# Moving the norm's weight into the second matrix of an MLP, and centring and scaling rows in one GpSimd instruction

## What is computed

```
x = attention(q, k, v)                      # 2304 x 512
h = x @ w_in                                # 2304 x 1024
sm = exp(h - max(h)) / (sum(exp(h - max(h))) + 1e-9)
solu = h * sm
mu = mean(solu);  var = mean((solu - mu) ** 2)
ln = (solu - mu) / sqrt(var + 1e-6) * g_ln  # g_ln: 1024 weights, one per column
y = ln @ w_out                              # 2304 x 512
out = softplus(y @ w_in2) @ w_out2
```

## Time and profile before

| | before |
|---|---|
| median of 3 executions | 927.47 us (927.47 to 928.46) |
| the profiled execution's own time | 928.05 us |
| its span in the profile | 926.2 us |
| PE busy | 900.5 us, 97% |
| DVE busy | 763.8 us, 82% |
| ACT busy | 499.7 us, 54% |
| POOL busy | 433.0 us, 47% |

### The profile page before, as it was taken

The page is one execution under the profiler, slowest core; times in us unless marked ns, Lnnn a source line. Parts: engine busy times, 40 slices in busy tenths (PEclk is TensorE's granted clock), DMA queues, the critical chain, the costliest instruction groups (busy, mean ns, idle before and its releaser), DMA issues.

```text
span 926.2 us, 15249 instructions
## 1 busy us (share of the span) xinstructions
PE 900.5 (97%) x5456; PEld 745.0 (80%) x5456; DVE 763.8 (82%) x1304; ACT 499.7 (54%) x936; POOL 433.0 (47%) x449
## 2 busy tenths in 40 slices
PE   7999999999999899999999899999999999999997
PEld 4666666666667698898999788899999999999995
DVE  6899998999874938448352799999999999999997
ACT  3777777778764624334342655445445545455543
POOL 3444444345652824123140555555556565556563
PEclk9999999999999999999999999999999999999999
DMA  6713413422210100000000720000000000000000
GB/s 168 204 29 77 104 41 65 103 73 61 65 47 1 42 6 1 1 1 1 1 12 1 233 74 1 35 1 1 35 1 1 35 1 1 34 0 0 34 0 35
DMA packets 29491, 37.58 MB, mean 41 GB/s; under 512 B 3696, under 2 KB 17520, under 8 KB 29424
## 3 DMA queue, kind: packets, MB, share of 16 engines
q1 hardware_dynamic: 29024, 36.42, 14.2%
q10 hardware_dynamic: 400, 0.30, 0.1%
HBM read 31.98 MB, written 4.72 MB: 40 GB/s over the span
## 4 chain that ended last, share of the span: by engine, by line
DVE 50%; PE 44%; issue 4%; ACT 1%; DMA 0%; POOL 0%; DVEq 0%; SPq 0%
DVE g L848 13%; PE y_ps L1042 11%; PE o_ps L978 9%; PE s_ps L940 9%; PE t_ps L951 7%; DVE g_hi L852 7%; DVE g L838 7%; DVE g_lo L854 6%; PE h_ps L909 5%; DVE g L841 5%; DVE x_lo L704 2%; DVE solu L805 1%; DVE ntop L709 1%; DVE st_top L791 1%; DVE ln_lo L767 1%
## 5 line engine op out<-in xcount | busy, mean ns | idle before, releaser
L451 POOL TENSOR_TENSOR w_lo<-w_raw,w_hi 128x512 fp32r<-128x512 f32 x96 | 131.8, 1374 | 161.2 <-ACT w_hi L631 159.1
L412 POOL TENSOR_SCALAR kept<-kept,inv 128x576 f32<-128x576 f32 x144 | 105.9, 751 | 137.4 <-DVE inv L741 137.4
L511 ACT ACTIVATE expd<-s_ps,ntop 128x576 f32<-128x576 f32 x144 | 104.7, 741 | 71.6 <-DVE ntop L709 71.6
L1018 PE MATMUL m_ps<-y_hi,w_lo 128*128 128x384 f32 x384 | 131.2, 342 | 0.0
L1018 PE MATMUL m_ps<-y_lo,w_hi 128*128 128x384 f32 x384 | 130.1, 339 | 0.0
L647 ACT ACTIVATE l<-u 128x384 f32<-128x384 f32 x96 | 50.4, 525 | 146.0 <-POOL u L459 146.0
L1018 PE MATMUL m_ps<-y_hi,w_hi 128*128 128x384 f32 x384 | 128.8, 335 | 0.0
L709 DVE TENSOR_REDUCE ntop<-s_ps 128x1 f32<-128x576 f32 x144 | 106.0, 755 | 23.6 <-PE s_ps L940 17.4
L459 POOL TENSOR_TENSOR u<-z,consts 128x384 f32<-128x384 f32 x96 | 105.8, 1102 | 41.7 <-ACT z L640 41.6
L1099 PE MATMUL f_ps<-w_hi,g_hi 128*128 128x512 f32 x288 | 115.8, 402 | 8.0 <-DVE g_lo L854 8.0
L848 DVE TENSOR_TENSOR g<-g,l 128x384 f32<-128x384 f32 x96 | 119.0, 1239 | 2.8
(11 more groups left out here) (85 smaller groups left out, 1803.7 us busy)
## 6 DMA issues: line engine op xcount, KB each, us to landing
q_sb<-q_t SPq DMA_DIRECT2D x28, 288.0 KB, 5.1
v_sb<-v_main SPq DMA_DIRECT2D x16, 256.0 KB, 3.2
stage<-w_in SPq DMA_DIRECT2D x16, 256.0 KB, 2.7
w_raw<-w_out SPq DMA_DIRECT2D x8, 512.0 KB, 6.5
out<-o_sb SPq DMA_DIRECT2D x5, 768.0 KB, 3.6
k_sb<-k_t SPq DMA_DIRECT2D x21, 144.0 KB, 4.6
stage<-w_in SPq DMA_DIRECT2D x4, 512.0 KB, 8.4
stage<-w_out SPq DMA_DIRECT2D x4, 512.0 KB, 3.6
```

Of the source, the lines that this page charges most:

```text
L412: nc.gpsimd.tensor_scalar(kept[:, tile % RING, :], kept[:, tile % RING, :], inv[:, group % 2, k:k + 1], 1.0, ALU.mult, ALU.mult).then_inc( ...
L451: nc.gpsimd.tensor_tensor(w4[1][:, n % 2, :], w4_raw[:, n % F2, :], f32(w4[0][:, n % 2, :]), ALU.subtract).then_inc(w4lo_made, 1)
L1018: last = nc.tensor.matmul(m_ps[n % 4][:, 0:GC], w[:, k, (n % F2) * P:(n % F2 + 1) * P], y[odd][:, k, :], start=(k == 0 and m == 0), stop=( ...
```

## The change

The norm's weight `g_ln` no longer multiplies the rows of `ln` but the rows of `w2`, once. It is loaded early as 128 x 8 numbers, with weight 128k + p in partition p and column k. In the doubles 72 to 75 of attention, the last ones, ACT multiplies each of the eight row blocks of `w2` in its `stage` slot by its column (`w2_scale`), before it takes the high part. In the first MLP DVE's instruction that made `(solu - mu) * gain` (L820) goes, and POOL's multiplication by `st_rstd` becomes one instruction with two per-partition scalars: `(solu + nmean) * rstd`. As POOL now reads `solu` itself, DVE waits before it writes a `solu` buffer until POOL has read the tile two before, and POOL waits for PE's transposes before it writes `ln`. POOL's loop over tiles is written out. The full diff:

```diff
@@ tensors
+        gain = sb("gain", [P, F1])
...
-        gain = sb("gain", [P, DFF1], where=phase)
@@ sync
                 sp.dma_start(staged(n)[0], staged_source(n)).then_inc(stage_in[n], 16)
+            sp.dma_start(gain[:, :], gain_d.rearrange("(k p) -> p k", p=P),
+                         allow_slow_non_contiguous=True).then_inc(gain_in, 16)
             for unit in range(2, UNITS):
...
-            sp.dma_start(gain[:, :], gain_d.partition_broadcast(P)).then_inc(gain_in, 16)
@@ gpsimd, norm
                 pool.wait_ge(rstd_made, tile + 1)
-                pool.wait_ge(z_made, tile + 1)
-                nc.gpsimd.tensor_tensor(ln[:, slot, :], ln[:, slot, :],
-                                        st["rstd"][:, col].broadcast_to([P, DFF1]), ALU.mult).then_inc(ln_made, 1)
+                pool.wait_ge(mean_made, tile + 1)
+
+                wait(pool, lt_made, tile - 1)
+                nc.gpsimd.tensor_scalar(ln[:, slot, :], solu[:, slot, :], st["nmean"][:, col], st["rstd"][:, col],
+                                        ALU.add, ALU.mult).then_inc(ln_made, 1)
...
-            three_parts(pool, MT, 6, norm, MT // 6)
+            for tile in range(MT):
+                norm(tile // 6, tile % 6)
@@ scalar
                 act.wait_ge(stage_in[n % STAGES], 16 * (n // STAGES + 1))
+                if C <= n < C + F1 // 2:
+                    act.wait_ge(w2_scaled, 2 * (n - C) + 2)
                 nc.scalar.copy(hi, src).then_inc(w_hi, 1)
+
+            def w2_scale(n):
+
+                src, hi, lo = staged(n)
+                act.wait_ge(stage_in[n % STAGES], 16 * (n // STAGES + 1))
+                act.wait_ge(gain_in, 16)
+                for a in range(2):
+                    m = 2 * (n - C) + a
+                    nc.scalar.activation(src[:, a, :], src[:, a, :], ACT.Copy, scale=gain[:, m:m + 1]
+                                         ).then_inc(w2_scaled, 1)
...
                     w1_high(v - 54)
+                if DOUBLES <= v < DOUBLES + F1 // 2:
+                    w2_scale(C + v - DOUBLES)
@@ vector, mlp1
                     dve.wait_ge(hinv_made, tile + 1)
+
+                    wait(dve, ln_made, tile - 1)
                     nc.vector.scalar_tensor_tensor(out=solu[:, slot, :], in0=h_ps[slot][:, :],
...
-                if within(tile, MT):
-                    dve.wait_ge(mean_made, tile + 1)
-
-                    wait(dve, lt_made, tile - 1)
-                    if isinstance(tile, int) and tile == 0:
-                        dve.wait_ge(gain_in, 16)
-                    nc.vector.scalar_tensor_tensor(out=ln[:, slot, :], in0=solu[:, slot, :],
-                                                   scalar=st["nmean"][:, col], in1=gain[:, :],
-                                                   op0=ALU.add, op1=ALU.mult).then_inc(z_made, 1)
```

More of the change, by code:

```diff
@@ L147, in build @@
         st = {n: sb("st_" + n, [P, 2], where=phase) for n in names.split()}
-        first_words = 2 * 2 * C * P + 7 * DFF1 + 2 * len(st)
+        first_words = 2 * 2 * C * P + 6 * DFF1 + 2 * len(st)
         sb("gap1", [P, SCORE_WORDS - first_words], where=phase)
@@ L216, in build @@
         e1_made, ese_made, hinv_made = sem("e1_made"), sem("ese_made"), sem("hinv_made")
-        solu_made, mean_made, z_made = sem("solu_made"), sem("mean_made"), sem("z_made")
+        solu_made, mean_made = sem("solu_made"), sem("mean_made")
+        w2_scaled = sem("w2_scaled")
         sq_made, msq_made = sem("sq_made"), sem("msq_made")
```

## The result

| | before | after |
|---|---|---|
| median | 927.47 us (927.03 to 928.46, 6 runs) | 922.61 us (921.91 to 924.36, 6 runs) |
| ratio, 95% interval | | 0.9946 [0.9936, 0.9956] |
| profiled execution, its span | 928.05, 926.2 | 922.69, 920.9 |
| DVE busy | 763.8 us | 732.0 us |
| POOL busy | 433.0 us | 411.4 us |

The change makes the kernel 0.54% faster, 5.0 us by the ratio. The profiled executions differ by 5.36 us, where the sum of the prediction was 5.28. DVE is busy 32 us less, and a sixth of that comes out as time. Of the 32 us, 23.3 are the pass that is gone, and 11.3 are waiting time: the 18 `x_lo` take 16.5 us where they took 27.8, as they wait less for POOL. In the rest of the kernel DVE is busy some 3 us longer.

A forecast was written before the change was run, and what follows sets the result against it. PE's waits for DVE's `ln_lo` in the first MLP, from a DVE-ACT-POOL loop slower than PE's step, were the bound. 3.39 + 1.89 = 5.28 us off 927.47 gave 922.2, range 921.0 to 925.0 (forecast's own 921.3 to 923.2).

The forecast's parts named there:

- The waits, not the busy time, are the prize: First MLP: PE's losses waiting for `ln_lo` go, 3.39 us in the early tiles and 1.89 us in three steady groups.
- The loop: First MLP's early tiles, `st_nmean` to `st_nmean` over DVE, ACT and POOL: 7.57 falls to 6.05 us, under PE's 6.47.
- POOL's new instruction: First MLP: the 1024-column `ln` with two per-partition scalars takes 1.20 us, against 1.89 for the old form.
- `st_msq`: First MLP, POOL: without DVE's `ln` pass it takes 0.19 us, not 1.02, freeing 0.83 us in the loop.
- Steady groups: First MLP, three later groups of three tiles: DVE's chain starts about 0.9 us earlier, 0.55 needed, saving 1.89 us.
- ACT's scalings: End of attention: eight of 0.7 us, 5.6 in all, fit ACT's gaps at cost 0, 0.8 spare in the last.
- The load of the weight: 1024 single numbers, issued at about 25 us and read at 274, take 4.7 us over 16 engines; cost 0.
- The new waits and the written-out loop of POOL: First MLP: what DVE and POOL newly wait for is over some 6 us earlier; more code, one branch less; cost 0.
- One collision: Rival, last of four early tiles: `x_lo` misses its turn behind POOL's 2.84 us low part; 924.2 us; chance 0.09.
- the triple one: Rival, first MLP: the same port collision in three early tiles, loop 8.9 against 7.57 us; 929.5 us; chance 0.04.
- Second MLP shifted as a whole: Second MLP: starts when the last y is complete, with the same order and gaps, so it only moves forward; 0.
- the slow-POOL rival: Rival, first MLP: POOL's new `ln` takes 1.6 us or more; at 1.89 PE loses 1.1, giving 923.3; chance 0.11.

The follow-up runs named there:

- the two halves: Two runs, e1_pool_form (POOL's new form without removing DVE's pass) and e2_pass_gone (the pass removed with POOL's old form): 923.38 and 924.3 us.
- e2_pass_gone: Changed kernel with POOL's old two-tensor multiplication on `solu`, centring left out, DVE's pass still gone: 924.3 us, ratio 0.9957 to the old kernel.
- e7_scale_alone: Old kernel with only ACT's eight scalings added, by 1.0 and without a load: 927.7 us against 927.9, ratio 1.0.
- e3_scale_twice: Changed kernel with each of ACT's eight scalings done twice, first by 1.0: 924.52 us, ratio 0.9962 to the old kernel.
- e5_two_pieces: Old kernel with POOL's multiplication for `ln` cut into two pieces of 512 columns: 923.72 us against 927.9, ratio 0.9954.
- e4_ln_sooner: Changed kernel without POOL's division by 1024 and epsilon, so that `ln` comes sooner: 923.48 us, ratio 0.9948 to the old kernel.
- e1_pool_form: Old kernel with POOL's multiplication taking one per-partition scalar and its tile loop written out, DVE's pass kept: 923.38 us against 927.95, ratio 0.9951.

## Why the prediction was right

922.2 was predicted, 922.61 measured, within the forecast's own range. By its steps:

- **The waits, not the busy time, are the prize.** 3.39 + 1.89 = 5.28 us. Measured: 3.38 in the early part, three groups of three tiles shorter by 0.64 each (36.73 to 36.09), and the last steps of the second MLP begin 5.36 us sooner (917.05 to 911.69), of which 0.07 is there before the first MLP starts: 5.29. So the sum was right by its terms, and the median's 4.86 differs from it by no more than runs of one kernel differ.
- **The loop.** 6.05 worked out, 6.07 measured; the two halves, 6.80 and 6.74 worked out, 6.81 and 6.73 measured. The experiments show that once PE waits it goes at the loop's pace; how much of the early part is lost depends also on when the first tile is late (e2_pass_gone).
- **POOL's new instruction.** 1.20 estimated from the rows of the same form, 1.20 measured (18 instructions, mean 1204 ns). The rate of 1.8 cycles an element, by the Trainium skill, page "GPSIMD Engine Reference", section 3.1, had made an estimate of 1.54 us; the measurement decides against it here.
- **`st_msq`** back at 0.19 us in all 18 tiles (mean 192 ns): right.
- **Steady groups.** `x_lo` starts 0.89 us after PE's step (351.11 after 350.22), before 1.21; 0.3 sooner had been read. `st_nmean` then comes 1.10 us earlier in the step (354.03 after 350.22, before 358.59 after 353.68), where 0.9 had been read.
- **ACT's scalings.** Cost 0: right, shown by e7_scale_alone; the copies behind the second pair came 0.1 us late, where a few tenths had been allowed. The spare room is 1.20 us and not 0.8, mostly since four take 2.56 and not 2.8; e3_scale_twice shows what lies beyond it.
- **The load of the weight.** 9.2 us until it had landed, not 4.7. The step was mis-sized by half, and it had over 200 us of cover: cost 0.
- **The new waits and the written-out loop of POOL,** each put at 0. After's list of waits of the first MLP shows no wait of DVE for POOL's `ln` and none of POOL's `ln` for the transposes. For the loop's 0 no row was given, and no run tests it alone; e5_two_pieces gains 3.74 us without it.
- **One collision (924.2) and the triple one (929.5).** Neither came. The margin worked out, 0.3 to 0.9 us, was 0.98 in the first tile looked at (`x_lo` asks 2.93 after `st_nmean`, `ln` ends 3.91 after) and 0.42 in the next (3.49 and 3.91). It was a real rival: with `ln` 0.6 us sooner it happened at the place named. Its price was set too high, about 2 us for the 1.03 that the first projection lost, in part as 2.84 includes POOL's own waiting.
- **Second MLP shifted as a whole:** right here, and luckier than it looked. e4_ln_sooner shows that its first dozen steps can fall into another order of port grants and move by 3 us; I had named that as what could make the prediction wrong, for all 96 steps, and gave it no chance of its own. The granted clock falls at the same two places of the second MLP in before and in after, and from its first product to the last matmul they take the same time (518.39 to 923.07 and 513.06 to 917.70), so it cancels.
- **Not foreseen:** that the slow-POOL rival (1.89 us) would lose 1.70 in the early part, not 1.1; its time would have been 923.9 and not 923.3.

## What to carry to other kernels

Close the loop before you count work: a pass that is taken from a busy engine is worth only what a loop over several engines exceeds the pace of the engine behind it, and two edits that each shorten that loop don't add. Where DVE and POOL share operands in SBUF, read the length of each hold and who asks first. A shorter or a divided POOL instruction gave as much as a removed DVE pass or more (4.64, 3.74 and 3.55 us), and a change that moves an instruction by half a microsecond can lose a turn of 2.4. And look for the cheap form elsewhere: a tensor operand that is only a broadcast number cost POOL 1.6 times as much, and changing it in 96 steps of the second MLP gave more than the change under study, though about half of that came through PE's clock.

## What the runs showed of the hardware

- On POOL a pass with scalars as operands is much faster than one that reads a broadcast number as a second tensor: 1024 columns 1.13 to 1.20 us against 1.89, 384 columns 0.51 against 0.83 in the shortest of the 96 instructions each. The mean over the 96 steps is 802 against 1101 ns.
- A waiting DVE instruction gets the port at the boundary between two POOL instructions that follow each other without a gap, and POOL's next instruction shows the wait in its own duration (2.85 for 2.40, 1.49 for 1.04). The DVE subtraction of 512 columns ends 0.52 to 0.58 us after the POOL instruction that held it, in before, after, e1_pool_form, e4_ln_sooner and e5_two_pieces.
- After a wait of 2.57 us in the last steps, PE's granted clock fell to its lower level (1.2 of 2.4 GHz) in after and not in e2_pass_gone, where PE had waited 2.56 us at the same place. The views by stretch, of after and then of e2_pass_gone:

```profile
912.00:918.00 6.00, 5.70 (x18) 4.12 (x16) 3.10 (x7) 0.59 (x1) 0.00 (x0) 0.72 0.04 16
```

```profile
914.00:920.00 6.00, 4.44 (x18) 2.96 (x17) 3.57 (x7) 0.59 (x1) 0.00 (x0) 1.00 0.18 65
```

The 18 matmuls took longer in one, and the end came 9.2 us after the start of step 94 against 8.3. Runs of one kernel differ too: of the twelve of before beside e1 to e4 the two with a mean clock of 1.0 took 927.00 and 927.07 us and the one with 0.992 took 929.75, though one with 0.998 took 930.30. So single spans of these kernels carry about 1 us that their edits don't explain, and the comparisons above go by medians and by the starts of steps. What decides whether the clock falls there stays open.
